# The convolution of a fused convolution and two MLPs, moved to another step of the block, with its copies on ScalarE and the split of x put ahead of a residue

## The reference

```python
# x (2, 4096, 192), weight (8, 7): causal depthwise convolution, one softmaxed kernel for each of 8 heads
w = exp(weight - max); w = w / (sum(w) + 1e-9)
c[b, s, h, :] = sum_k w[h, k] * x_pad[b, s + k, h, :]         # 24 channels a head
# MLP 1 on all 8192 tokens, 192 -> 2048 -> 192
h1 = c @ w_in1;  y = maximum(0.01 * h1, h1) @ w_out1
# MLP 2, 192 -> 2048 -> 192, with a rational activation
h = y @ w_in2
g = (a0 + a1 h + a2 h^2 + a3 h^3) / (1 + |b0| |h| + |b1| h^2 + 1e-6)
out = g @ w_out2                                               # float32 throughout
```

## Time and profile before

| | us |
|---|---|
| median of 3 runs | 1347.91 (1347.9 to 1348.41) |
| profiled execution, device time | 1347.41 |
| its span | 1345.5 |
| PE busy | 1264.7 (94%) |
| DVE busy | 1059.5 (79%) |
| ACT busy | 1033.0 (77%) |
| POOL busy | 618.7 (46%) |

### The profile page before, as it was taken

How to read it: one execution, slowest core, us unless ns; L and a number is a source line. 1 busy time by engine, 2 the same in 40 slices (tenths; PEclk the granted TensorE clock), 3 DMA queues, 4 the chain that set the end, 5 groups by cost and what they waited for, 6 DMA issues and landing times.

```text
span 1345.5 us, 14840 instructions
## 1 busy us (share of the span) xinstructions
PE 1264.7 (94%) x5724; PEld 1027.6 (76%) x5724; DVE 1059.5 (79%) x945; ACT 1033.0 (77%) x1027; POOL 618.7 (46%) x265
## 2 busy tenths in 40 slices
PE   7989999999999999999999999999999999999774
PEld 6768787877878787787877878787787878778553
DVE  3667878878788788878878787877878788787896
ACT  4677777878777877887877877787787788788763
POOL 0034454544545445445445454454544544545664
PEclk8999999999999999999999999999999999999887
DMA  6200000000000000000000000000000000000000
GB/s 191 78 1 13 0 25 1 12 13 1 24 1 25 0 12 13 1 25 0 13 13 13 13 0 25 1 12 14 12 13 1 25 1 13 1 1 12 0 12 12
DMA packets 25093, 21.74 MB, mean 16 GB/s; under 512 B 2909, under 2 KB 23997, under 8 KB 25023
## 3 DMA queue, kind: packets, MB, share of 16 engines
q1 hardware_dynamic: 25023, 20.80, 5.3%
HBM read 14.49 MB, written 6.30 MB: 15 GB/s over the span
## 4 chain that ended last, share of the span: by engine, by line
PE 58%; DVE 20%; ACT 11%; POOL 5%; issue 4%; DMA 1%; POOLq 0%; SPq 0%; DVEq 0%; ACTq 0%
PE h L611 29%; DVE den L508 6%; PE acc L621 5%; PE acc L630 5%; PE acc L631 5%; PE acc L623 5%; PE acc L622 5%; DVE hi L496 5%; DVE den L502 5%; POOL den L313 4%; ACT rec L394 4%; ACT rec L397 2%; ACT hi L389 2%; ACT h L385 2%; PE h L576 2%
## 5 line engine op out<-in xcount | busy, mean ns | idle before, releaser
L313 POOL TENSOR_TENSOR den<-den,rec 128x1024 f32<-128x1024 f32 x128 | 313.2, 2447 | 706.3 <-DVE den L508 415.6
L611 PE MATMUL h<-xs,wa 128*128 128x512 f32 x2520 | 612.5, 395 | 25.3 <-DVE xs L475 15.0
L611 PEld LDWEIGHTS h<-xs,wa 128*128 128x128 f32 x2520 | 471.5, 189 | 145.5 <-DVE xs L475 19.9
L319 POOL TENSOR_TENSOR lo<-den,rec 128x1024 fp32r<-128x1024 f32 x128 | 308.6, 2411 | 11.0 <-DVE den L508 11.0
L496 DVE SCALAR_TENSOR_TENSOR hi<-pol,coef_a,rec 128x1024 fp32r<-128x1024 f32 x128 | 164.3, 1283 | 94.6 <-issue 48.3
L621 PE MATMUL acc<-hi,wb 128*128 128x512 f32 x512 | 206.4, 403 | 20.0 <-DVE xs L489 19.9
L522 DVE TENSOR_TENSOR lo<-h,hi 128x1024 fp32r<-128x1024 f32 x128 | 156.3, 1221 | 86.8 <-ACT hi L389 86.8
L630 PE MATMUL acc<-lo,wb 128*128 128x512 f32 x512 | 201.5, 394 | 20.1 <-POOL lo L319 20.1
L363 ACT ACTIVATE rec<-h 128x1024 f32<-128x1024 f32 x124 | 127.3, 1027 | 111.6 <-PE h L611 111.6
L385 ACT ACTIVATE h<-h 128x1024 f32<-128x1024 f32 x128 | 129.3, 1010 | 98.6 <-PE h L611 98.6
L623 PE MATMUL acc<-hi,wb 128*128 128x512 f32 x512 | 201.0, 393 | 0.0
(11 more groups left out here) (85 smaller groups left out, 899.6 us busy)
## 6 DMA issues: line engine op xcount, KB each, us to landing
out<-edge SPq DMA_DIRECT2D x16, 384.0 KB, 2.6
x_tok<-in_x SPq DMA_DIRECT2D x64, 82.5 KB
rec<-in_moe_w_out SPq DMA_DIRECT2D x4, 384.0 KB, 4.6
x_tok<-in_x SPq DMA_DIRECT2D x16, 78.0 KB
pol<-in_moe_w_out SPq DMA_DIRECT2D x3, 384.0 KB, 3.9
pol<-in_moe_w_in SPq DMA_DIRECT2D x2, 512.0 KB, 6.6
den<-in_moe_w_in SPq DMA_DIRECT2D x2, 512.0 KB, 4.5
rec<-in_moe_w_in SPq DMA_DIRECT2D x4, 256.0 KB, 5.4
```

The costliest lines, as they stand in the source:

```text
L313: nc.gpsimd.tensor_tensor(den[k][:, :], den[k][:, :], rec[n % RECS][:, :], ALU.mult).then_inc(s_den, 1)
L319: nc.gpsimd.tensor_tensor(lo2[k][:, :], den[k][:, :], rec[(n - 1) % RECS][:, :], ALU.mult).then_inc(s_lo2, 1)
L611: last = T.matmul(dst[:, half, :], lhs, xs[m][:, part, :], start=(j == 0), stop=(j == 4))
```

## The change

The convolution of blocks 2 and on goes from phase 4 to phase 7, the step behind the one that transposes the block before it. Since it is then seven steps ahead of its own transposition, conv_sb gets a buffer of its own, and so does out_tok. Both halves of the convolution's result are copied by ACT for those blocks. Block 1 is convolved in step -4 as before and block 2 in step -1 (before: step 4). In phase 7 ACT's L375 moves behind L381. In phase 6 DVE does `residue(n-1)`, which used to end step n-1, behind `split_xt`.

```diff
-CONV_AT, XT_AT, SPLIT_AT, FOLD_AT, OUT_AT = 4, 6, 7, 1, 2
+CONV_AT, XT_AT, SPLIT_AT, FOLD_AT, OUT_AT = 7, 6, 7, 1, 2
+CONV_1 = -4
-        edge = sb("edge", [P, CTILES * D])
-        conv_sb = edge[0:CT, :].rearrange("p (t d) -> p t d", t=CTILES)
+        conv_sb = sb("conv_sb", [CT, CTILES, D])
-        out_tok = edge[:, 0:SUB * D].rearrange("p (t d) -> p t d", t=SUB)
+        out_tok = sb("out_tok", [P, SUB, D])
         def conv_block(n):
-            return (n + LEAD + XT_AT - CONV_AT) // STEPS
+            if n < -1:
+                return 1 if n == CONV_1 else -1
+            return (n + LEAD + STEPS + XT_AT - CONV_AT) // STEPS if n % STEPS == CONV_AT else -1
 # ScalarE
             def copy_conv(c):
                 act.wait_ge(s_conv, c + 1)
-                wait(act, s_stored, 16 * (c - 2))
                 nc.scalar.activation(conv_dst(0), conv_ps(c, 0), ACT.Copy).then_inc(s_conv_a, 1)
+                if c > 1:
+                    nc.scalar.activation(conv_dst(1), conv_ps(c, 1), ACT.Copy).then_inc(s_conv_b, 1)
...
-                if runs(n, PAIRS):
-                    act.wait_ge(s_abs, n + 1)
-                    wait(act, s_lo2, n - 1)
-                    nc.scalar.activation(den[k][:, :], r, ACT.Identity, ...).then_inc(s_slope, 1)
-                if phase == CONV_AT and runs(conv_block(n), BLOCKS):
+                if runs(n, PAIRS) and phase != CONV_AT:
+                    slope(n)
+                if runs(conv_block(n), BLOCKS):
                     copy_conv(conv_block(n))
                 if runs(n, PAIRS):
                     wait(act, s_res, n - 1)
                     nc.scalar.activation(pol[k][:, :], hidden_2_all(n), ACT.Identity, ...).then_inc(s_lin, 1)
+                    if phase == CONV_AT:
+                        slope(n)
 # VectorE
                 if phase == XT_AT and n > -LEAD and runs(m0 // STEPS, BLOCKS):
                     split_xt(m0 // STEPS)
+                if phase == XT_AT and runs(n - 1, PAIRS):
+                    residue(n - 1)
                 if phase == OUT_AT and runs(o0, BLOCKS):
                     out_sums(o0)
-                if phase == CONV_AT and runs(conv_block(n), BLOCKS):
-                    copy_conv(conv_block(n))
+                if conv_block(n) == 1:
+                    copy_conv(1)
...
                 if runs(n, PAIRS):
                     quotient_hi(n)
                     product(n)
-                    residue(n)
+                    if phase != XT_AT - 1:
+                        residue(n)
 # TensorE
-                convolves = phase == CONV_AT and runs(conv_block(n), BLOCKS)
+                convolves = runs(conv_block(n), BLOCKS)
...
                         if convolves and conv_block(n) > 1:
                             pe.wait_ge(s_conv_a, conv_block(n) + 1)
-                            pe.wait_ge(s_conv_v, conv_block(n) + 1)
+                            pe.wait_ge(s_conv_b, conv_block(n) - 1)
```

More of the change, by code:

```diff
@@ L104, in conv_mlp_mlp @@
         one = sb("one", [P, 1])
-        conv_row = edge
+        conv_row = conv_sb[:, :, :].rearrange("p a c -> p (a c)")
         out_row = out_cm[:, :, :].rearrange("p a c -> p (a c)")
@@ L148, in conv_mlp_mlp @@
         s_conv_v = sem("conv_copied_dve")
+        s_conv_b = sem("conv_rest_copied_act")
         s_xt = sem("xt_in_psum")
@@ L371, in step @@
                                              ACT.Copy).then_inc(s_ot_copy, 1)
-                if runs(n, PAIRS):
-                    act.wait_ge(s_abs, n + 1)
-                    wait(act, s_lo2, n - 1)
-                    nc.scalar.activation(den[k][:, :], r, ACT.Identity, scale=coef_b[:, 1:2],
-                                         bias=coef_b[:, 0:1]).then_inc(s_slope, 1)
-                if phase == CONV_AT and runs(conv_block(n), BLOCKS):
+                if runs(n, PAIRS) and phase != CONV_AT:
+                    slope(n)
+                if runs(conv_block(n), BLOCKS):
                     copy_conv(conv_block(n))
@@ L399, in step, with slope @@
                     out_leaves(o0)
+            def slope(n):
+                act.wait_ge(s_abs, n + 1)
+                wait(act, s_lo2, n - 1)
+                nc.scalar.activation(den[n % 2][:, :], rec[n % RECS][:, :], ACT.Identity, scale=coef_b[:, 1:2],
+                                     bias=coef_b[:, 0:1]).then_inc(s_slope, 1)
             def out_leaves(c):
@@ L441, in copy_conv @@
                 dve.wait_ge(s_conv, c + 1)
-                wait(dve, s_stored, 16 * (c - 2))
                 V.tensor_copy(conv_dst(1), conv_ps(c, 1)).then_inc(s_conv_v, 1)
@@ L583, in transpose_x @@
                 pe.wait_ge(s_conv_a, c + 1)
-                pe.wait_ge(s_conv_v, c + 1)
+                if c > 1:
+                    pe.wait_ge(s_conv_b, c - 1)
+                else:
+                    pe.wait_ge(s_conv_v, c + 1)
                 for j, first in enumerate(CFIRST):
```

## The result

The changed kernel takes 1311.95 us (median of 4 runs, 1311.49 to 1312.23); the kernel before, beside it, 1348.11. The ratio is 0.9731 with a 95% interval of 0.9714 to 0.9748, so it is 2.7% faster. The forecast was 1314 with a range of 1304 to 1329. The profiled execution took 1311.49, with a span of 1309.4 in place of 1345.5.

What follows compares the result with a forecast made beforehand. PE, busy 94% of the span, was taken as the bound. 15.8 + 28.5 - 5.9 - 4.3 = 34.1 us off 1347.4 gave 1313.3; with 0.5 for the median, 1314 us, range 1304 to 1329.

Steps and rivals of the forecast that it cites:

- Phase 4, 28.5 us: Phase 4, steps 4 to 108: without the convolution the step falls to the 9.07 floor; 28.5 us gained.
- Phase 6, 15.8 us: Phase 6: with DVE's split of x ahead of the residue, the wait for L475 goes; 15.8 us gained.
- Phase 7, nothing: Phase 7: the convolution's 1.57 us fit into 1.90 of PE waiting; the step stays at 10.94, costing nothing.
- What the late slope costs, 5.9 us: Phase 2: the later slope of phase 7 delays the residue and PE waits; 5.9 us lost, bounds 0 to 15.6.
- POOL starts L313 at 8.15, ends at 10.6: Phase 7, times from the step's start: POOL's L313 waits for the late slope L375, then lasts 2.45.
- The round of 8.8: Steps after phase 7: a round of the residue's chain lasts 8.8, so each step gives back some 0.3 of lateness.
- The prologue, 4.3 us: Step -1: block 2's convolution and copies precede up(0), so step 0 starts at 79.2, not 74.91; 4.3 us lost.
- The tail: Steps 119 and 127: the slope is 1.2 later; up to 1.3 us later at the end, left out of the sum.
- the split is held: Rival in phase 6: L475 and L478 come no earlier, the step stays 11.16, 15.8 lost, 1330 us; chance 0.11.
- phase 7 pays: Rival in phase 7: DVE chain or copies late by one place, the convolution costs 21, 1335 us; chance 0.09.
- The rival on the other side: Rival, slower than before: phase 7's late L508 delays L514 and L516 of phase 0; 1351 us at 3.3; chance 0.05.
- The covered case: Rival: the late slope and the prologue are covered, at most 2 lost, 1304 to 1308 us; chance 0.17.

Runs made afterwards that it cites:

- Experiment 1: The changed kernel with the residue back at the end of step n-1, so the convolution in phase 7 alone (also written e1): 1320.56 us.
- experiments 6 and 7: The changed kernel with the convolution of blocks 3 to 15 issued twice, 1334.4 us, and with half of its heads left out, 1308.24 us.
- e8: The changed kernel with half of the convolution's heads left out for blocks 3 to 15 (the second of experiments 6 and 7): 1308.24 us.
- e4: The changed kernel with the slope of phase 7 between the two copies and the numerator's first term: 1311.4 us.
- e5: The changed kernel with the second half of the convolution's result copied by DVE, behind the split of x in phase 7: 1359.44 us.
- e2: The kernel before with the split of x ahead of the residue in phase 6, the convolution left in phase 4: 1330.99 us.

## Why the prediction was right, and where its reasons were not

- **Phase 4, 28.5 us**: as forecast, 9.07 in each block.
- **Phase 6, 15.8 us**: 16.4 measured; the 0.6 more come mostly from one step of before that was 0.4 longer than its like. But the split is not its only cause. Experiment 1 shows that moving the convolution alone gives 0.54 of the 1.13 a block. I had taken 11.16 as phase 6's length with or without a convolution in phase 4. The sum came out because both parts are in the change.
- **Phase 7, nothing**: right to 0.03 us, and experiments 6 and 7 show it by both signs. The sentence that the gain of phase 6 is what makes it possible was wrong: seen from its own start, phase 7's DVE chain lies the same with and without it (10.97 in e1). The prediction's own layout has this in it: the chain and the step's start both move by some 1.14, so the distance between them does not.
- **What the late slope costs, 5.9 us**: size near (4.6 measured), cause wrong. The step of the prediction that failed is "POOL starts L313 at 8.15, ends at 10.6", taken as what L394 waits for. L394 stands behind the leaky ReLU on ACT, which waits for `up(0)`, and in a step with extra work `up(0)` is one `down(1)` and one convolution later. By the prediction's own numbers this path ends at 10.6 too (`up(0)` over at 626.75 - 618.23 = 8.5, then L385 and L389), so the number hid the mistake. Measured, POOL is done at 10.10, since it starts at 7.70 in place of 8.15, and L398 starts at 10.67, behind L393. That the figure came out is luck: by the path that I named alone L398 would start at about 10.13, and phase 2 would cost next to nothing (e8); e4 separated the two. What follows from there (residue 5.9 into phase 0, some 0.3 given back in each step, a late L534) is in the trace: the residue ends at 313.18 - 307.30 = 5.9 and starts at 4.60, 4.20 and 3.93 in phases 0, 1 and 2. The round of 8.8 is stated with L508 in it twice: the terms as listed add up to 9.97, and to 8.7 without the second L508.
- **The prologue, 4.3 us**: 4.45, by the chain that was laid out, as the three waits ahead of 69.94, 73.00 and 79.02 show.
- **The tail**: left out of the sum. From step 118 on the trace is 102.1 long, 101.9 before. The later slope did not cost the 1.3 us that the prediction allowed there. In step 127 POOL's multiply starts later beside DVE (1287.61) and lasts 2.84 in place of 3.38, so that it ends 3.44 us after the start of the product in both kernels.
- **The rivals**: "the split is held" and "phase 7 pays" did not happen. The rival on the other side (the lateness reaches the numerator) stayed in its margin. e5 shows the nearest thing to it, by another way: one late copy turns the whole change into a loss. The covered case is stated as 1304 to 1308; its terms give 1304 to 1306. The two new buffers were not tried by themselves; the waits that went with them ended nothing in the trace before, and e2, with the old buffer, has the whole gain of phase 6.

The sum was 34.1, the span fell by 36.1: 0.6 more in phase 6, 1.3 less lost in phase 2 and 0.3 ahead of step -4, less some 0.15 each in the prologue and the tail.

## What to carry to other kernels

Where the busiest engine waits at a fixed place in a period, independent work of the same length can be moved there at no cost in that step; lay both engines out from the start of that step to see how much fits, and follow what it delays there: here `up(0)` came later in its step, and 4.6 us of waiting came out three steps on. Where an engine runs its instructions in the order written, as here, an instruction that another engine waits for goes ahead of one whose reader has slack, and the same edit is worth trying wherever a short wait is left (phase 2 gave 4.4 us more by the medians, 5.1 by the steps). When two paths end close together, a right number does not tell which one binds: shorten one and look.

## What the runs showed of the hardware

In 11 of the 13 blocks of e5 a PE gap of 2.65 us was followed by a granted clock of 0.50 (1.2 GHz), for some 3.4 us in five of them and some 6.8 us in the six last; in the two others the same gap was followed by nothing, and the runs do not show why. The kernel before, whose gaps that recur in every block are at most 1.35 us, had a granted clock of 1.00 (2.4 GHz) from 150 to 1200 us. I had not counted this in e5: a gap cost 1.6 us more by it in the first case and 2.9 in the second.
